# The first eight attention units: scores in banks of their own, computed two units ahead, with fills of 512 columns of zeros

## The chip, the cores and the metric

The kernel runs on one core of a Trainium2 chip. The metric is the device time of one execution in microseconds (us), the median of several runs; lower is better. The engines are TensorE (PE, with its weight loads as PEld), VectorE (DVE), ScalarE (ACT), GpSimd (POOL) and SyncE (SP), which here only issues DMAs.

## What is computed

Three layers follow one another. The first is local attention over 4 batches, 8 heads, 768 tokens and a head size of 64; the other two are gated feed-forward layers over the 3072 resulting rows of 512 numbers.

```python
for c in range(nc):                       # 24 chunks of 32 queries
    k_full = np.concatenate([mem_k, k_ctx], axis=2)   # 8 + up to 56 keys
    v_full = np.concatenate([mem_v, v_ctx], axis=2)
    scores = scale * np.matmul(q_c, k_full.transpose(0, 1, 3, 2))
    scores = scores - np.max(scores, axis=-1, keepdims=True)
    a = np.exp(scores)
    a = a / (np.sum(a, axis=-1, keepdims=True) + 1e-09)
    out[:, :, c_start:c_end] = np.matmul(a, v_full)
...
x = (1/(1+np.exp(-(x @ w_gate))) * (x @ w_val)) @ w_out       # 512 -> 1536 -> 512
h = x @ w_in                                                  # 512 -> 2048
g = (a0 + a1*h + a2*h**2 + a3*h**3) / (1 + |b0|*|h| + |b1|*h**2 + 1e-6)
y = g @ w_out
```

## The kernel before, in words

**Units.** The 768 tokens of a sequence are cut into 6 tiles of 128. A tile of one batch is a unit: 128 queries of 8 heads. The first eight units (two tiles of four batches) are computed before any feed-forward work exists. The later units are mixed into feed-forward products and are not touched by the change, apart from names.

**One unit g.** Five steps follow each other, and each waits for the one before:

1. `scores(g)`, TensorE: 32 small matmuls of q and k into two of the four banks of `ps_h` (`ps_att[g % 2]`).
2. `softmax(g)`, VectorE: a row maximum, and scores minus maximum into `probs`. `exp_scores(g)`, ScalarE, in place. `normalize(g)`, VectorE: (in the first tile a small memset,) row sum, plus 1e-9, reciprocal, multiplication.
3. `turn(g)`, TensorE: four transposes, again into `ps_att[g % 2]`; `copy_turned(g)`, ScalarE, to `probs_t`.
4. `weigh_values(g)`, TensorE: 32 small matmuls with v, again into `ps_att[g % 2]`.
5. `stage_x(g)`, ScalarE: out of `ps_att[g % 2]` to `x_raw`, and the semaphore `x_staged`.

All three matmul steps of a unit use the same two banks, so `scores(g)` waits for `stage_x(g-2)`. Every fp32 matmul is two matmul records in the trace; the fp32r matmuls of the feed-forward part are one.

**Order.** All order is written out by hand, engine by engine. `attention(first, fill)` goes through pairs of units; `fill(p, place)` or `at(p, place)` puts other work between the steps. On TensorE this other work is `warm_up(n)`, n products of the identity with itself into a bank of `ps_y` that nobody reads, and towards the end `early_product(c, m)`, the first products of the feed-forward layer. On ScalarE and VectorE it is the splitting of weights (`split_w(c, i)`) and of x (`split_x`) into a high and a low part for fp32r products, each time the high part on ScalarE first, then the low part on VectorE. VectorE also makes `token_sum(T1..T4, g)`, differences of parts of x. After unit 7, `last_operands` makes the last sums and splits: `token_sum(T3, 0)`, `(T4, 0)`, three splits and `split_w(1, 3)`, then `token_sum(T1, 1)` and `(T2, 1)`, which need the last staging.

**Loads.** SyncE issues them in order. `load_qk(g)` (q 256 KB, k 368 KB) writes one of two buffers and waits for `scores(g-2)`; `load_v(g)` (512 KB) waits for `weigh_values(g-2)`; `load_raw(c)` (512 KB) brings gate and value weights, from which GpSimd makes four sums. A load that waits holds back all loads behind it.

## Time and profile before

| | before |
|---|---|
| median of 3 runs | 1165.22 us (1165.1 to 1166.02) |
| the profiled execution | 1163.57 us |
| its span | 1161.6 us |
| TensorE busy | 1145.8 us (99%) |
| VectorE busy | 926.5 us (80%) |
| ScalarE busy | 750.9 us (65%) |
| GpSimd busy | 123.3 us (11%) |

The durations in the text come from the profiled execution. Its own time is 1.97 us more than its span, and 1.65 us under the median. "Busy" of TensorE counts its fills too, and a matmul record lasts longer than the time until the next one may follow.

### The profile page before, as it was taken

What the parts mean: (1) busy time and instruction counts of PE and PEld (TensorE: products, weight loads), DVE (VectorE), ACT (ScalarE), POOL (GpSimd) and SP (SyncE); (2) the same over time, 40 slices, a digit from 0 to 9 for tenths busy, and PEclk for the clock granted to TensorE, in tenths of its full rate; (3) what the DMA queues carried; (4) which work ended last, traced back from release to release, by engine and by line L of the source; (5) the groups of instructions that cost most, each with busy time, mean ns of one, the idle gap of its engine ahead of it and who ended that gap; (6) DMA issues with size and microseconds to landing.
All of it is one profiled execution on the core that took longest, in us unless ns stands there. A gap on an engine that the chain in (4) does not pass through costs nothing.

```text
span 1161.6 us, 20825 instructions
## 1 busy us (share of the span) xinstructions
PE 1145.8 (99%) x7954; PEld 942.8 (81%) x7954; DVE 926.5 (80%) x1419; ACT 750.9 (65%) x1224; POOL 123.3 (11%) x150
## 2 busy tenths in 40 slices
PE   7899999999999999999999999999999999999998
PEld 6788887778888777888888888888888888888887
DVE  5886767776676777777667998988988988988987
ACT  3665555455555555555556877877877877877875
POOL 2052230012233001223100000000000000000000
PEclk9999999999999999999999999999999999999999
DMA  7511412742141374323137100200200200200100
GB/s 261 165 64 55 163 55 95 230 149 91 60 157 55 100 234 158 109 86 105 46 129 264 42 1 1 73 1 1 72 0 0 72 0 0 72 0 0 37 1 37
DMA packets 40720, 94.05 MB, mean 81 GB/s; under 512 B 4288, under 2 KB 4288, under 8 KB 40640
## 3 DMA queue, kind: packets, MB, share of 16 engines
q1 hardware_dynamic: 40640, 92.95, 23.7%
q8 instruction: 54, 0.88, 0.3%
q14 instruction: 26, 0.21, 0.1%
HBM read 80.35 MB, written 12.58 MB: 80 GB/s over the span
## 4 chain that ended last, share of the span: by engine, by line
PE 94%; DVE 3%; issue 1%; DMA 1%; ACT 0%; SPq 0%; POOL 0%; ACTq 0%; POOLq 0%; DVEq 0%
PE ps_h L1253 9%; PE ps_h L1255 9%; PE ps_h L1260 9%; PE ps_h L1417 7%; PE ps_h L1412 7%; PE ps_h L1413 7%; PE ps_y L1456 7%; PE ps_y L1452 7%; PE ps_y L1450 7%; PE ps_y L1332 5%; PE ps_y L1337 5%; PE ps_y L1333 4%; PE ps_h L1235 2%; PE ps_h L1211 2%; PE ps_y L1321 1%
## 5 line engine op out<-in xcount | busy, mean ns | idle before, releaser
L1253 PE MATMUL ps_h<-xop,wop 128*128 128x512 f32 x484 | 188.3, 389 | 0.0
L1255 PE MATMUL ps_h<-xop,wop 128*128 128x512 f32 x484 | 188.3, 389 | 0.0
L1412 PE MATMUL ps_h<-x_split,weights 128*128 128x512 f32 x384 | 149.4, 389 | 0.0
L1413 PE MATMUL ps_h<-x_split,weights 128*128 128x512 f32 x384 | 149.4, 389 | 0.0
L1260 PE MATMUL ps_h<-xop,wop 128*128 128x512 f32 x484 | 149.0, 389 | 0.0
L1450 PE MATMUL ps_y<-weights,hid 128*128 128x512 f32 x360 | 140.0, 389 | 0.0
L1452 PE MATMUL ps_y<-weights,hid 128*128 128x512 f32 x360 | 140.0, 389 | 0.0
L878 DVE TENSOR_TENSOR wop<-rawp,wop 128x448 fp32r<-128x448 f32 x144 | 91.1, 661 | 32.7 <-ACT wop L494 32.7
L757 ACT ACTIVATE tmp<-ps_h 128x512 f32<-128x512 f32 x96 | 57.2, 595 | 92.4 <-PE ps_h L1417 92.4
L899 DVE TENSOR_TENSOR x_raw<-ps_h,probs_t 128x512 f32<-128x512 f32 x70 | 48.1, 687 | 79.6 <-PE ps_h L1260 79.3
L1332 PE MATMUL ps_y<-hid,wout 128*128 128x512 f32 x264 | 105.7, 400 | 0.6 <-DVE stage_h L930 0.3
L1253 PEld LDWEIGHTS ps_h<-xop,wop 128*128 128x128 f32 x484 | 90.8, 188 | 18.9
L1260 PEld LDWEIGHTS ps_h<-xop,wop 128*128 128x128 f32 x484 | 90.9, 188 | 18.9
L1255 PEld LDWEIGHTS ps_h<-xop,wop 128*128 128x128 f32 x484 | 90.8, 188 | 18.8
L1333 PE MATMUL ps_y<-hid,wout 128*128 128x512 f32 x264 | 103.1, 391 | 0.0
L1417 PE MATMUL ps_h<-x_split,weights 128*128 128x512 f32 x384 | 102.6, 389 | 0.0
L1456 PE MATMUL ps_y<-weights,hid 128*128 128x512 f32 x360 | 96.2, 389 | 0.0
L1130 DVE TENSOR_TENSOR tmp<-tmp 128x512 f32<-128x512 f32 x96 | 66.1, 689 | 30.8 <-ACT tmp L760 30.7
L535 ACT ACTIVATE hid<-x_raw 128x512 fp32r<-128x512 f32 x72 | 45.4, 631 | 63.4 <-DVE x_raw L913 63.4
L1413 PEld LDWEIGHTS ps_h<-x_split,weights 128*128 128x128 f32 x384 | 72.1, 188 | 15.0
L1417 PEld LDWEIGHTS ps_h<-x_split,weights 128*128 128x128 f32 x384 | 72.1, 188 | 14.9
L1412 PEld LDWEIGHTS ps_h<-x_split,weights 128*128 128x128 f32 x384 | 72.0, 188 | 14.9
(103 smaller groups left out, 2277.9 us busy)
## 6 DMA issues: line engine op xcount, KB each, us to landing
rawp<-wgv_l SPq DMA_DIRECT2D x36, 512.0 KB, 3.8
oraw<-wo_l SPq DMA_DIRECT2D x72, 256.0 KB, 3.9
unit<-v_l SPq DMA_DIRECT2D x24, 512.0 KB, 4.5
unit<-k_l SPq DMA_DIRECT2D x24, 368.0 KB, 4.2
unit<-q_l SPq DMA_DIRECT2D x24, 256.0 KB, 3.4
x_stage<-y_dram SPq DMA_DIRECT2D x6, 1024.0 KB, 5.7
out<-stage SPq DMA_DIRECT2D x24, 256.0 KB, 2.3
braw<-wb_l SPq DMA_DIRECT2D x11, 512.0 KB, 5.6
```

Source lines behind the costliest of these rows:

```text
L878: nc.vector.tensor_tensor(wop[:, c % 2, 1, cols], rawp[:, c % 2, 256 + 448 * i:256 + 448 * (i + 1)], wop[:, c % 2, 0, cols].bitcast(F32), ...
L1253: nc.tensor.matmul(dst, w_h[k], xop[:, m, 0, k, :], start=first and k == 0, stop=False, skip_group_check=True)
L1255: nc.tensor.matmul(dst, w_l[k], xop[:, m, 0, k, :], start=False, stop=False, skip_group_check=True)
L1260: last = nc.tensor.matmul(dst, w_h[k], xop[:, m, 1, k, :], start=False, stop=k == 1, skip_group_check=True)
L1332: nc.tensor.matmul(ps_y[:, m, :], w_at(0, m), h[0], start=f == 0, stop=False)
L1333: nc.tensor.matmul(ps_y[:, m, :], w_at(1, m), h[0], start=False, stop=False)
L1412: nc.tensor.matmul(dst, lhs(c, 0), x_split[:, 0, c, :], start=(c == 0), stop=False)
L1413: nc.tensor.matmul(dst, lhs(c, 1), x_split[:, 0, c, :], start=False, stop=False)
L1417: last = nc.tensor.matmul(dst, lhs(c, 0), x_split[:, 1, c, :], start=False, stop=(c == KT - 1))
L1450: nc.tensor.matmul(ps_y[:, m, :], hid_b(i, 0)[:, P * m:P * (m + 1)], wb_at(i, 1, 0), start=(i == 0), stop=False)
L1452: nc.tensor.matmul(ps_y[:, m, :], hid_b(i, 0)[:, P * m:P * (m + 1)], wb_at(i, 1, 1), start=False, stop=False)
L1456: nc.tensor.matmul(ps_y[:, m, :], hid_b(i, 1)[:, P * m:P * (m + 1)], wb_at(i, 1, 0), start=False, stop=False)
```

## The change

Only the first eight units are concerned.

- Their scores go to `ps_y` (`ps_first`), which is free at that time. Turned probabilities and outputs stay in `ps_att`. `scores(g)` of these units waits for `shifted` (the subtraction of unit g-2) instead of `x_staged`.
- Scores are computed two units ahead: `first_attention` replaces `attention(0, ...)` on TensorE, ScalarE and VectorE. Row maxima get a tile of their own (`row_maxima`), since the maximum of unit g+2 is now taken near the row sums of unit g.
- A fill is one product of the identity with 512 columns of zeros (`wide_fill`) into a bank of `ps_att` that holds nothing then, instead of `warm_up(3)` of 128 columns into `ps_y`. GpSimd zeroes the tile of zeros after the identity.
- SyncE asks for q and k of unit 2 right after those two of units 0 and 1 and V of unit 0, and so on.
- `split_w` and `split_x` have new places in the list.

```diff
-WARM = 3
+WARM = 6
...
+        ps_first = [ps_y[:, 0:2, 0:256], ps_y[:, 2:4, 0:256]]
...
-            for g in range(2):
+            load_qk(0)
+            load_qk(1)
+            load_v(0)
+            load_qk(2)
+            load_v(1)
+            load_qk(3)
+            load_raw(0)
+            for g in range(4, UNITS):
                 load_qk(g)
-            for g in range(2):
-                load_v(g)
-            load_raw(0)
-            load_qk(2)
-            for g in range(3, UNITS):
-                load_qk(g)
-                if g == 3:
+                load_v(g - 2)
+                if g == 4:
                     load_raw(1)
-                load_v(g - 1)
+            load_v(UNITS - 2)
             load_v(UNITS - 1)
```

VectorE, in place of `attention(0, at_start)`:

```diff
+            def first_attention():
+                softmax(0)
+                softmax(1)
+                for g in range(UNITS):
+                    normalize(g)
+                    if g == 2:
+                        split_w(0, 0)
+                    elif g == 3:
+                        split_w(0, 1)
+                    elif g == 4:
+                        split_w(0, 3)
+                        split_x(0, B11)
+                    elif g == 5:
+                        split_x(0, B21)
+                    elif g == 6:
+                        token_sum(0, T1, 0)
+                        token_sum(0, T2, 0)
+                        split_w(1, 2)
+                    if g + 2 < UNITS:
+                        softmax(g + 2)
+                    if g == 3:
+                        split_w(0, 2)
+                    elif g == 4:
+                        split_w(1, 0)
+                    elif g == 5:
+                        split_w(1, 1)
```

ScalarE, in place of the same call:

```diff
+                exp_scores(0)
+                exp_scores(1)
+                for g in range(UNITS):
+                    copy_turned(g)
+                    if g + 2 < UNITS:
+                        exp_scores(g + 2)
...
+                    stage_x(g)
+                    if g == 1:
+                        split_w(0, 0)
+                    elif g == 2:
+                        split_w(0, 1)
+                        split_w(0, 2)
+                    elif g == 3:
+                        split_x(0, B11)
+                        split_w(0, 3)
+                        split_w(1, 0)
```

TensorE:

```diff
                 if n >= 2:
-                    pe.wait_ge(x_staged, g - 1)
+                    if s:
+                        pe.wait_ge(x_staged, g - 1)
+                    else:
+                        pe.wait_ge(shifted, g - 1)
...
+            def wide_fill(b):
+                nc.tensor.matmul(ps_h[:, 2 * b, :], ident[:], zeros[:], start=True, stop=True)
...
+            def first_attention():
+                scores(0)
+                pe.wait_ge(ident_done, 3)
+                wide_fill(0)
+                scores(1)
+                for g in range(UNITS):
+                    if 1 <= g < UNITS - 2:
+                        scores(g + 2)
+                    turn(g)
+                    if g:
+                        pe.wait_ge(x_staged, g)
+                    if g == UNITS - 1:
+                        early_product(1, M1)
+                    else:
+                        wide_fill((g + 1) % 2)
+                    weigh_values(g)
+                    if g == 0:
+                        scores(2)
+                    elif g == UNITS - 2:
+                        early_product(0, M1)
+                        early_product(0, M2)
+                    else:
+                        wide_fill((g + 1) % 2)
+                early_product(1, M2)
```

**TensorE, the start of the program.** `ident` by `ident` is a warm-up, `unit` 32x64 are scores, `ident,probs` are the turns, `probs_t,unit` is the weighing of values. Before:

```order
L1242 MATMUL ps_y<-ident 128x128 x6
L1211 MATMUL ps_h<-unit 32x64 x32
L1242 MATMUL ps_y<-ident 128x128 x3
L1211 MATMUL ps_h<-unit 32x64 x32
L1242 MATMUL ps_y<-ident 128x128 x2
L1221 MATMUL ps_h<-ident,probs 128x128 x4
L1242 MATMUL ps_y<-ident 128x128 x3
L1235 MATMUL ps_h<-probs_t,unit 64x32 x32
L1242 MATMUL ps_y<-ident 128x128 x3
L1211 MATMUL ps_h<-unit 32x64 x32
L1221 MATMUL ps_h<-ident,probs 128x128 x4
L1242 MATMUL ps_y<-ident 128x128 x3
```

And now, where `zeros,ident` is a wide fill:

```order
L1235 MATMUL ps_y<-unit 32x64 x32
L1272 MATMUL ps_h<-zeros,ident 128x512
L1235 MATMUL ps_y<-unit 32x64 x32
L1247 MATMUL ps_h<-ident,probs 128x128 x4
L1272 MATMUL ps_h<-zeros,ident 128x512
L1261 MATMUL ps_h<-probs_t,unit 64x32 x32
L1235 MATMUL ps_y<-unit 32x64 x64
L1247 MATMUL ps_h<-ident,probs 128x128 x4
L1272 MATMUL ps_h<-zeros,ident 128x512
L1261 MATMUL ps_h<-probs_t,unit 64x32 x32
L1272 MATMUL ps_h<-zeros,ident 128x512
```

Scores of unit 2 stand behind the weighing of unit 0 in both, but those of unit 3 now follow them at once, and from there on two sets of scores are ahead of the turn. Each product of these rows is two records in the trace, a turn is one.

**VectorE, the start of the program.** A reduce of `ps` with a subtraction is a softmax, the memset to the multiplication is a normalize. Before:

```order
L817 TENSOR_REDUCE row_stats<-ps_h 128x8
L820 TENSOR_TENSOR probs<-ps_h,row_stats 128x2x4x64
L830 MEMSET probs 32x8x16
L835 TENSOR_REDUCE row_stats<-probs 128x8
L837 TENSOR_SCALAR row_stats<-row_stats 128x8
L839 RECIPROCAL row_stats<-row_stats 128x8
L841 TENSOR_TENSOR probs<-probs,row_stats 128x2x4x64
L817 TENSOR_REDUCE row_stats<-ps_h 128x8
L820 TENSOR_TENSOR probs<-ps_h,row_stats 128x2x4x64
L830 MEMSET probs 32x8x16
```

And now:

```order
L827 TENSOR_REDUCE row_maxima<-ps_y 128x8
L830 TENSOR_TENSOR probs<-ps_y,row_maxima 128x2x4x64
L827 TENSOR_REDUCE row_maxima<-ps_y 128x8
L830 TENSOR_TENSOR probs<-ps_y,row_maxima 128x2x4x64
L840 MEMSET probs 32x8x16
L845 TENSOR_REDUCE row_stats<-probs 128x8
L847 TENSOR_SCALAR row_stats<-row_stats 128x8
L849 RECIPROCAL row_stats<-row_stats 128x8
L851 TENSOR_TENSOR probs<-probs,row_stats 128x2x4x64
L827 TENSOR_REDUCE row_maxima<-ps_y 128x8
L830 TENSOR_TENSOR probs<-ps_y,row_maxima 128x2x4x64
```

The softmax of unit 1 moved ahead of normalize(0), and the softmax of unit 2 ahead of normalize(1).

**SyncE, the loads, with what each waits for.** From the load of q of unit 1 on. Before:

```order
L262 DMA unit<-q_l 128x512
L263 DMA unit<-k_l 128x736
L268 DMA unit<-v_l 128x1024 x2
L274 DMA rawp<-wgv_l 128x1024
L262 DMA unit<-q_l 128x512 [waits scores_done]
L263 DMA unit<-k_l 128x736
L262 DMA unit<-q_l 128x512 [waits scores_done]
L263 DMA unit<-k_l 128x736
L274 DMA rawp<-wgv_l 128x1024
L268 DMA unit<-v_l 128x1024 [waits pv_done]
```

And now:

```order
L266 DMA unit<-q_l 128x512
L267 DMA unit<-k_l 128x736
L272 DMA unit<-v_l 128x1024
L266 DMA unit<-q_l 128x512 [waits scores_done]
L267 DMA unit<-k_l 128x736
L272 DMA unit<-v_l 128x1024
L266 DMA unit<-q_l 128x512 [waits scores_done]
L267 DMA unit<-k_l 128x736
L278 DMA rawp<-wgv_l 128x1024
L266 DMA unit<-q_l 128x512 [waits scores_done]
L267 DMA unit<-k_l 128x736
```

V of unit 1 and the first weights (`rawp`) now stand behind a load that waits for scores; before, they were issued at once.

## Rows read from the trace of the kernel before

**Rows 1.** Windows view, core 0: length, then PE, PEld, DVE, ACT, POOL busy, clock, DMA, GB/s

```profile
5.76:54.11 48.35, 40.47 (x1110) 34.73 (x1110) 39.21 (x72) 23.19 (x40) 6.18 (x8) 0.96 0.64 220
...
57.00:1161.00 1104.00, 1099.12 (x6761) 902.63 (x6759) 885.08 (x1344) 723.87 (x1179) 116.41 (x136) 1.00 0.22 74
...
20.28:23.70 3.42, 3.42 (x77) 3.13 (x75) 2.54 (x4) 1.92 (x5) 0.47 (x1) 0.52 0.71 215
```

**Rows 2.** Waits of VectorE, 5.7 to 54.2 us: total us, times, longest

```profile
DVE row_stats L817 <- PE ps_h L1211: 10.6, 5, 5.8
DVE probs L830 <- ACT probs L456: 2.0, 4, 0.7
DVE wop L878 <- ACT wop L494: 0.7, 1, 0.7
DVE row_stats L835 <- ACT probs L456: 0.3, 2, 0.2
```

**Rows 3.** Timeline of VectorE: start, us, engine, line, operation, idle before

```profile
5.76 0.69 DVE L817 TENSOR_REDUCE row_stats<-ps_h 128x8 f32<-128x512 f32 x1 [5.76 <-PE ps_h L1211]
6.49 0.69 DVE L820 TENSOR_TENSOR probs<-ps_h,row_stats 128x512 f32<-128x512 f32 x1
7.92 0.17 DVE L830 MEMSET probs<- 32x128 f32 x1 [0.74 <-ACT probs L456]
...
9.28 0.69 DVE L841 TENSOR_TENSOR probs<-probs,row_stats 128x512 f32<-128x512 f32 x1
...
53.42 0.69 DVE L858 TENSOR_TENSOR t_raw<-x_raw 128x512 f32<-128x512 f32 x1
```

**Rows 4.** Timeline of TensorE, units 1 and 2

```profile
7.69 0.85 PE L1211 MATMUL ps_h<-unit 64*32 64x64 f32 x64 [0.59 <-DMA unit<-k_l]
...
10.03 0.66 PE L1221 MATMUL ps_h<-ident,probs 128*128 128x128 f32 x4 [0.84 <-DVE probs L841]
...
11.42 1.13 PE L1235 MATMUL ps_h<-probs_t,unit 64*64 64x32 f32 x62
13.61 0.30 PE L1235 MATMUL ps_h<-probs_t,unit 64*64 64x32 f32 x2 [1.07 <-issue]
13.84 0.94 PE L1242 MATMUL ps_y<-ident 128*128 128x128 f32 x6
14.71 0.86 PE L1211 MATMUL ps_h<-unit 64*32 64x64 f32 x64
15.50 0.66 PE L1221 MATMUL ps_h<-ident,probs 128*128 128x128 f32 x4
15.99 0.83 PE L1242 MATMUL ps_y<-ident 128*128 128x128 f32 x6
16.89 0.89 PE L1235 MATMUL ps_h<-probs_t,unit 64*64 64x32 f32 x45
19.16 0.54 PE L1235 MATMUL ps_h<-probs_t,unit 64*64 64x32 f32 x19 [1.38 <-issue]
```

**Rows 5.** Waits of TensorE, 4 to 54.5 us

```profile
PE ps_h L1235 <- issue: 3.0, 3, 1.4
```

**Rows 6.** Timeline of TensorE in the stretch of low clock

```profile
21.60 1.11 PE L1221 MATMUL ps_h<-ident,probs 128*128 128x128 f32 x4
22.51 1.48 PE L1242 MATMUL ps_y<-ident 128*128 128x128 f32 x6
```

**Rows 7.** Timeline of TensorE, unit 6 and first products

```profile
44.81 1.14 PE L1235 MATMUL ps_h<-probs_t,unit 64*64 64x32 f32 x64
...
46.44 0.40 PE L1253 MATMUL ps_y<-xop,wop 128*128 128x512 f32 x1
46.67 0.39 PE L1255 MATMUL ps_y<-xop,wop 128*128 128x512 f32 x1
```

**Rows 8.** Page, DMA queues: packets, MB, share of 16 engines

```profile
q8 instruction: 54, 0.88, 0.3%
```

**Rows 9.** Groups of ScalarE by line and shape, 4 to 54.5 us

```profile
L472 ACT ACTIVATE x_raw<-ps_h 128x512 f32<-128x512 f32 x8 | 4.8, 595 | 8.9 <-PE ps_h L1235 8.9
```

More of the change, by code:

```diff
@@ L114, in build @@
         ps_att = [ps_h[:, 0:2, 0:256], ps_h[:, 2:4, 0:256]]
+        ps_first = [ps_y[:, 0:2, 0:256], ps_y[:, 2:4, 0:256]]
         probs = [probs_all[:, b, :].rearrange("p (h s k) -> p h s k", h=HP, s=2) for b in range(2)]
         probs_t = [probs_t_all[:, b, :].rearrange("p (h n) -> p h n", h=HP) for b in range(2)]
-        row = [row_stats[:, b].rearrange("p (s h) -> p s h", s=2) for b in range(2)]
+        row, row_max = [[x[:, b].rearrange("p (s h) -> p s h", s=2) for b in range(2)] for x in (row_stats, row_maxima)]
         NQC, NKC, NVC = HP * P, CT * HP * KEYS, CT * HP * D
@@ L432, in _ @@
                                     pattern=[[-1, P]], channel_multiplier=1).then_inc(ident_done, 1)
+            nc.gpsimd.memset(zeros[:], 0.0).then_inc(ident_done, 1)
             def weight_sums(c):
@@ L814, in softmax @@
                 b = g % 2
-                sc = ps_att[b].rearrange("p s (h k) -> p s h k", k=KEYS)
+                sc = (ps_first if g < UNITS else ps_att)[b].rearrange("p s (h k) -> p s h k", k=KEYS)
                 dve.wait_ge(scores_done, g + 1)
-                nc.vector.tensor_reduce(row[b], sc, AX.X, ALU.max).then_inc(max_done, 1)
+                nc.vector.tensor_reduce(row_max[b], sc, AX.X, ALU.max).then_inc(max_done, 1)
                 dve.wait_ge(max_done, g + 1)
@@ L820, in softmax @@
                 nc.vector.tensor_tensor(probs[b].rearrange("p h s k -> p s h k"), sc,
-                                        row[b].unsqueeze(3).to_broadcast([P, 2, HP, KEYS]),
+                                        row_max[b].unsqueeze(3).to_broadcast([P, 2, HP, KEYS]),
                                         ALU.subtract).then_inc(shifted, 1)
@@ L1196, in scores @@
                 b, s, n = g % 2, g // UNITS, g % UNITS
+                dst = (ps_att if s else ps_first)[b]
                 pe.wait_ge(qk_loaded[b], 32 * (g // 2 + 1))
                 if n >= 2:
[L1199 removed]
+                    if s:
+                        pe.wait_ge(x_staged, g - 1)
+                    else:
+                        pe.wait_ge(shifted, g - 1)
                 elif s and n == 0:
@@ L1238, in weigh_values, with warm_up @@
                 last.then_inc(pv_done, 1)
-            def warm_up(products):
+            def warm_up(products, b=0):
                 for _ in range(products):
-                    nc.tensor.matmul(ps_y[:, 3, 0:P], ident[:], ident[:], start=True, stop=True)
+                    nc.tensor.matmul(ps_att[b][:, 0, 0:P], ident[:], ident[:], start=True, stop=True)
+            def wide_fill(b):
+                nc.tensor.matmul(ps_h[:, 2 * b, :], ident[:], zeros[:], start=True, stop=True)
             def product(c, m):
@@ L1345, in attention @@
                     scores(a)
-                    if b == 1:
-                        warm_up(WARM)
-                        scores(b)
                     if p:
@@ L1354, in attention @@
                     fill(p, 1)
-                    if b > 1:
-                        scores(b)
+                    scores(b)
                     if p == 0:
@@ L1366, in attention, with first_attention @@
                 fill(UNITS // 2, 1)
-            def fill_first(p, place):
-                if (p, place) == (3, 4):
-                    early_product(0, M1)
-                    early_product(0, M2)
-                elif (p, place) == (4, 0):
-                    early_product(1, M1)
-                elif (p, place) == (4, 1):
-                    warm_up(WARM)
-                    early_product(1, M2)
-                elif place != 2:
-                    warm_up(1 if p == 0 and place < 2 else WARM)
+            def first_attention():
+                scores(0)
[8 more added lines that the diff above has]
+                        pe.wait_ge(x_staged, g)
+                    if g == UNITS - 1:
+                        early_product(1, M1)
[10 more added lines that the diff above has]
+                early_product(1, M2)
             pe.wait_ge(ident_done, 2)
-            warm_up(2 * WARM)
-            attention(0, fill_first)
+            warm_up(WARM)
+            first_attention()
             for s in range(NS):
```

67 lines of the change are left out of this document (19 added, 48 removed).

## The prediction, made blind

> **What bounds the kernel now.** The windows view comes first. From 57 us to 1161 us TensorE is busy for 1099.12 of 1104 us [rows 1], so nothing there is shortened by this change. What the change touches lies ahead of that point; it can only move the moment at which the dense part begins.
>
> In the first 57 us I looked for an engine that does the same work before and after and sits on the path. That is VectorE. Its work from the first row maximum (5.76) to the last sum that the late operands need, `token_sum(T2,1)` (starts 53.42, 0.69 long, so it ends at 54.11) [rows 3], is the same set of instructions in both kernels; only their order differs. ScalarE's split of that sum, and behind it the dense product chain, hang on it. So the question is: how long does VectorE stand idle in this stretch, before and after?
>
> Before: the stretch is 48.35 us and VectorE is busy for 39.21 [rows 1]. Its waits are 10.6 less the 5.8 ahead of the first instruction, 2.0, 0.7 and 0.3, that is 7.8 us [rows 2]; the remaining 1.3 us are the small gaps between instructions. The largest part, 4.8, is waiting for scores, so TensorE is late. It is late for a reason of its own: it stops inside runs of matmuls that wait for no other engine. Weighing the values alone stops three times, 3.0 us, as "issue" [rows 5]. Between two such stops (13.61 and 19.16) stand 2+6+64+4+6+45 = 127 matmul records [rows 4]; with their weight loads 254 instructions, with two semaphore instructions 256. The instruction queue moved 54 packets with 0.88 MB, 16.3 KB each [rows 8], which is 256 instructions of 64 bytes. I read this as instruction fetch: blocks of 256 come one at a time, and late when TensorE eats small matmuls fast. The block from 13.61 to 19.16 took 5.5 us, 1.38 of them standing still [rows 4].
>
> **What the change does, part by part.** I go through VectorE's new order and add up its idle time.
>
> *Wait for the scores of unit 1.* VectorE now does two softmaxes first. It is done with the first at 6.49+0.69 = 7.18 [rows 3]. Scores of unit 1 used to start at 7.69, when their K had landed, and took 0.85 [rows 4], so VectorE would wait 1.4. V of unit 1 and the first weights, which shared the queues with this load, now go out behind a wait, so K should land earlier; with the fill ahead of the scores ending near 7.0 the wait is 0.7 at least. I take 0.9. What goes away is the wait for the exponential at the small memset, 2.0 us in four places [rows 2], since another softmax now stands between.
>
> *Wait for the scores of unit 2.* This is the largest term. VectorE does normalize(0), then softmax(2). TensorE does turn(0), fill, weigh(0), and only then scores(2). From the end of normalize: 0.05 until the turn; 1.39 from the start of the turn to the start of weighing (10.03 to 11.42) [rows 4]; weighing 1.14 with the tail of its last record, 1.07 until the next may follow [rows 7]; scores 0.86 [rows 4] and 0.03 until VectorE starts. Together 3.4 us, 3.3 to 3.6, in which VectorE has nothing to do. Before, normalize(1) filled that hole.
>
> *Fills.* An old one is three products, six records; a new one is one product of 512 columns, two records. Six records of 128 columns take 0.83, each following the last by some 0.11 [rows 4]. A record of 512 columns in the fp32r form follows by 0.23 (46.44 to 46.67) [rows 7]. So a new fill costs between 2 x 0.23 = 0.46, if each record passes its columns once, and 4 x 0.22 = 0.89, if an fp32 record costs twice its columns, as 0.11 against a quarter of 0.23 says. I take 0.89. The fill between turn and weighing is free either way: four turns of 0.11 and 0.89 make 1.33, under the 1.39 that the copy between them takes anyway. The one behind weighing costs its 0.89, 0.2 more than the old one.
>
> *Pace afterwards.* TensorE per unit: scores 0.79 (14.71 to 15.50) [rows 4], turn to weighing 1.39, weighing 1.07, fill 0.89, together 4.1. VectorE per unit: softmax 1.42, normalize 2.05 (7.92 to 9.97) [rows 3], so 3.5, and from unit 2 on some 8 us of splits and sums spread over five units. So VectorE is as slow as TensorE or slower, unless TensorE stops. A unit has 64+64+4+4 = 136 records (144 before), still about one fetch per unit. Counted on from the first stop of before, which stood behind record 222, blocks now end behind scores(4), in scores(5), (6) and (7), and in weigh(6). The stop behind scores(4) delays turn(2), and VectorE may not overwrite those probabilities before it: 1.3, about the 1.38 of the row. The next costs 0.3; the later ones fall while VectorE has splits to do. I take 1.6, with 0.3 (only the 0.3 is left) and 2.8 (twice a stop of 1.4) as bounds.
>
> *Splits.* split_w(0,0) on VectorE now stands behind normalize(2). ScalarE can deliver it at 1.39 + 1.14 + 0.05 + 0.60 for staging [rows 9] + 0.6 for its own half, 3.8 us behind the start of turn(1); VectorE wants it at 0.7+0.7+2.05 = 3.5. So it waits 0.3. The same holds for two more, one of them behind a longer split: 1.2 together, at least 0.5.
>
> *Tail.* turn(7) now stands behind weigh(6) and two products, twelve records at 0.23 (2.7 us), while its normalize is long done. The last staging then comes late for VectorE by 0.5, between 0 and 1.0.
>
> Sum: 0.9 + 3.4 + 1.6 + 1.2 + 0.5 = 7.6 us idle, against 7.8. What is gained late in the phase is paid for by the hole at its beginning.
>
> *Clock.* In the stretch 20.28 to 23.70 the granted clock was 0.52 [rows 1], that is the 1.2 GHz level; just before it TensorE had stood still for 1.38. At this level the turn took 1.11 and the fill 1.48 [rows 6], against 0.66 and 0.83 [rows 4]. In the new order TensorE stands still for longer than anywhere before: from about 7.9 to 11.6 ahead of turn(0), and some 2.8 us ahead of turn(1). If the clock falls there it costs 0.45 on the turn, part of 0.89 on the fill and 0.2 on weighing, 1.5 in all if it covers them. I take 0.9 for one fall that covers them in part, and 1.9 as the bound.
>
> The Trainium skill, "TensorE: Matmul & The Clock Gate" (Why this matters for your kernels), warns of idle gaps between bursts of matmuls, since they bring the lower clock back. This rule speaks against the change; the trace agrees as far as its one fall stands behind a stop.
>
> So idle is 8.5 against 7.8, and the dense part starts 0.8 later in round numbers (the terms are rounded to 0.1). The profiled execution took 1163.57 (1161.6 of span and 1.97 around it) and becomes 1164.4. The median of the runs shown is 1165.22, 1.65 above it, and I put the forecast on the median: **1166.0**. About 0.2% (2.3 us) is what a measurement of this kernel can tell from no change.
>
> **Rivals.**
> *Faster (0.17).* Fetches arrive while TensorE waits for normalize anyway, the clock stays up, and K of unit 1 lands early: idle 0.7 + 3.3 + 0.3 + 0.6 + 0.2 = 5.1, 2.7 less than before, 1162.5. For it speaks that the DMA engines are used for only 0.64 of the stretch [rows 1], so that a fetch need not queue. Against it: the hole of 3.3 stays in every case, and so the other terms must nearly vanish together.
> *Slower (0.27), the clock.* Place: turn(0) to weigh(0) and turn(1) to weigh(1), both behind 2.8 us or more in which TensorE has nothing to do. If the clock falls both times and covers both, that is 3.0 on top of 7.6, 2.8 later, 1168.0. It decides when both stretches run at 1.2 GHz; with one of them the time stays within 0.2%. Against it: TensorE stopped several times before, and the clock fell once.
> *The fills cost half (0.04).* With 0.46 each TensorE reaches the end of a block sooner and waits there longer, by about as much as it saves: 1165.6.
> *No fetch stops (0.05).* If a whole phase fitted into the instruction memory, the stops would be something else, tied to the old order, and could be gone: 8.5 less 1.6, 0.9 less than before, 1164.3.
> *The forecast (0.47).* Idle within 1.5 us of 8.5: 1164.5 to 1167.4.
>
> The Trainium skill, "Advanced Engine Details and Errata" (ISA Cache), gives lines of 16 KB, 256 instructions, as the packets here have, but 128 KB in all for TensorE. By that size fetches could run far ahead, as in the case without fetch stops; the stops inside runs of matmuls speak against it.
>
> **Range.** Low bounds together: 0.7+3.3+0.3+0.5+0 = 4.8, 3.0 less than before: 1162.2. High bounds: 1.4+3.6+2.8+1.2+1.0+1.9 = 11.9, 4.1 more: 1169.3. I take 1162.8 to 1169.0. Faster 0.17; within 0.2% 0.56 (the forecast, the cheap fills, no fetch stops); slower 0.27.
>
> **What would show it.** In the profile of the changed kernel VectorE's reduction of unit 2 waits 3.3 to 3.6 us for scores, that of unit 1 0.7 to 1.4; the two records of a wide fill follow each other by 0.44 at full clock; stops of TensorE stand 127 records apart, the first between scores(4) and turn(2); token_sum(T2,1) ends near 54.9. The prediction is wrong if the scores of unit 2 come before 14.0, if the stops vanish, or if TensorE stays at 1.2 GHz over several stretches.

## The result: 7 us slower

The changed kernel takes 1172.98 us (median of 6 runs, 1171.06 to 1176.52), the one before 1165.94 (6 runs, 1165.1 to 1167.1): a ratio of 1.0066, with an interval of 1.0053 to 1.0078, so 7.0 us more. A second session gave 1172.24 against 1165.38, 1.0053 [1.0033 to 1.0073]. The forecast was 1166.0, with 1169.0 as the upper end of its range. The profiled execution took 1173.7 us.

The windows view of the changed kernel, cut at VectorE's first row maximum and at the end of `token_sum(T2,1)` (length, then PE, PEld, DVE, ACT, POOL busy, clock, DMA share, GB/s):

```profile
5.83:61.14 55.31, 45.35 (x1044) 29.25 (x1044) 38.27 (x72) 23.19 (x40) 6.04 (x8) 0.81 0.59 198
61.14:1171.60 1110.46, 1102.31 (x6770) 905.00 (x6768) 886.41 (x1348) 726.33 (x1183) 117.25 (x136) 1.00 0.22 74
```

VectorE runs the same 72 instructions as before [rows 1], but the stretch is 55.31 us instead of 48.35, and it ends 7.03 later. What lies behind it, 1110.46, was 1107.49 in the single profile of before. Over the kernels of this study this second part lies between 1107.5 and 1113.1 in the profiled executions, 1107.5 to 1110.4 in the old order and 1108.1 to 1113.1 in the new one, so I take most of those 3.0 us for scatter, which isn't shown: the medians differ by 7.0, as the first part does, while these two profiled executions differ by 10.1.

Waits of VectorE in that stretch (total us, times, longest; the first line holds the 5.83 ahead of the stretch):

```profile
DVE row_maxima L827 <- PE ps_y L1235: 15.7, 5, 5.9
DVE wop L888 <- ACT wop L501: 3.4, 3, 1.9
DVE probs L830 <- PE ps_h L1247: 1.1, 2, 0.7
DVE x_raw L863 <- ACT x_raw L479: 0.7, 1, 0.7
DVE xop L880 <- ACT xop L491: 0.6, 1, 0.6
```

That is 9.9 + 3.4 + 1.1 + 0.7 + 0.6 = 15.7 us of waiting, against 7.8 [rows 2] and the 8.5 of the forecast. The wait for the exponential is gone, as expected. Where the new ones stand is in its timeline:

```profile
8.54 0.69 DVE L827 TENSOR_REDUCE row_maxima<-ps_y 128x8 f32<-128x512 f32 x1 [1.29 <-PE ps_y L1235]
17.86 0.69 DVE L827 TENSOR_REDUCE row_maxima<-ps_y 128x8 f32<-128x512 f32 x1 [5.89 <-PE ps_y L1235]
27.20 0.66 DVE L888 TENSOR_TENSOR wop<-rawp,wop 128x448 fp32r<-128x448 f32 x1 [1.92 <-ACT wop L501]
29.19 0.69 DVE L827 TENSOR_REDUCE row_maxima<-ps_y 128x8 f32<-128x512 f32 x1 [1.34 <-PE ps_y L1235]
35.52 0.69 DVE L827 TENSOR_REDUCE row_maxima<-ps_y 128x8 f32<-128x512 f32 x1 [1.38 <-PE ps_y L1235]
```

The largest part of the excess is in one row: the scores of unit 2 are waited for 5.89 us, where 3.3 to 3.6 were forecast. TensorE's timeline shows what it did meanwhile:

```profile
12.03 1.11 PE L1247 MATMUL ps_h<-ident,probs 128*128 128x128 f32 x4 [3.53 <-DVE probs L851]
12.94 1.92 PE L1272 MATMUL ps_h<-zeros,ident 128*128 128x512 f32 x2
14.78 1.93 PE L1261 MATMUL ps_h<-probs_t,unit 64*64 64x32 f32 x64
16.64 2.05 PE L1235 MATMUL ps_y<-unit 64*32 64x64 f32 x128
21.35 1.11 PE L1247 MATMUL ps_h<-ident,probs 128*128 128x128 f32 x4 [2.66 <-DVE probs L851]
22.26 1.91 PE L1272 MATMUL ps_h<-zeros,ident 128*128 128x512 f32 x2
```

It stood still for 3.53 us, and then turn, fill, weighing and scores ran at the lower clock: the turn takes the 1.11 of [rows 6], the weighing 1.86 to the next row instead of 1.07. The windows view gives the clock:

```profile
8.60:10.00 1.40, 0.00 (x0) 0.00 (x0) 1.37 (x3) 0.01 (x1) 0.00 (x0) 1.00 0.92 341
10.10:30.50 20.40, 15.81 (x339) 10.59 (x340) 9.73 (x21) 4.79 (x9) 6.04 (x8) 0.50 0.63 218
30.60:61.00 30.40, 27.00 (x639) 17.52 (x638) 25.40 (x47) 17.55 (x31) 0.00 (x0) 1.00 0.51 163
```

From 10.1 to 30.5 us, three units long, TensorE has the 1.2 GHz level (0.50), and before and behind it 2.4 GHz. It fell while TensorE stood still ahead of turn(0). Before, the low stretch was 3.4 us long [rows 1]. One of the prediction's own signs of being wrong is thus there: TensorE stays at 1.2 GHz over several steps and units.

In the low stretch TensorE has no stop for issue. Behind it there are three, 3.1 us together, inside `scores(5)`, `scores(6)` and, not shown, `scores(7)`:

```profile
33.34 0.77 PE L1235 MATMUL ps_y<-unit 64*32 64x64 f32 x55
35.14 0.32 PE L1235 MATMUL ps_y<-unit 64*32 64x64 f32 x9 [1.02 <-issue]
...
38.95 0.71 PE L1235 MATMUL ps_y<-unit 64*32 64x64 f32 x46
40.69 0.41 PE L1235 MATMUL ps_y<-unit 64*32 64x64 f32 x18 [1.02 <-issue]
```

### The profile page after: what moved, and what is told of

It is laid out like the page before. It is cut to its first block, busy times and chain, and to the rows that moved or that the text cites. A ratio compares the mean times of both kernels' runs of the same rounds, so it can differ in the third digit from the quotient of the medians.

```text
span 1171.6 us, 20696 instructions
## 1 busy us (share of the span) xinstructions
PE 1151.8 (98%) x7888; PEld 938.0 (80%) x7888; DVE 924.7 (79%) x1419; ACT 750.8 (64%) x1224; POOL 124.5 (11%) x151
## 4 chain that ended last, share of the span: by engine, by line
PE 94%; DVE 3%; DMA 1%; issue 1%; SPq 0%; ACT 0%; ACTq 0%; DVEq 0%
PE ps_h L1283 9%; PE ps_h L1285 9%; PE ps_h L1290 9%; PE ps_h L1457 7%; PE ps_h L1453 7%; PE ps_h L1452 7%; PE ps_y L1496 7%; PE ps_y L1492 7%; PE ps_y L1490 7%; PE ps_y L1362 5%; PE ps_y L1367 5%; PE ps_y L1363 4%; PE ps_h L1261 2%; PE ps_y L1351 1%; PE ps_h L1247 1%; PE ps_h L1235 1%
```

## Experiments

Each kernel ran several times beside the kernel before. The last four columns are in us and come from the one profiled execution. T2 is the start of `token_sum(T2,1)`. "Waits" are VectorE's, from its first row maximum to the end of that sum. "At 1.2" is the time at the lower clock ahead of T2. "Issue" is what TensorE's waits put down to issue from 4 us to the end of T2. A 0.001 of the ratio is 1.2 us.

| kernel | median us | ratio, interval | T2 | waits | at 1.2 | issue |
|---|---|---|---|---|---|---|
| before | 1165.94 | | 53.42 | 7.8 | 3.4 | 6.0 |
| changed | 1172.98 | 1.0066 [1.0053, 1.0078] | 60.45 | 15.7 | 20.5 | 3.1 |
| scores(2) early | 1169.59 | 1.0033 [1.0021, 1.0046] | 57.26 | 12.1 | 6.8 | 5.7 |
| fills in the waits | 1169.75 | 1.0034 [1.0021, 1.0047] | 57.14 | 11.6 | 0 | 5.9 |
| narrow fills | 1169.22 | 1.0022 [1.0007, 1.0037] | 56.33 | 11.9 | 13.7 | 0.5 |
| before, wide fills | 1166.91 | 1.0005 [0.9989, 1.002] | 55.80 | 9.9 | 3.4 | 6.2 |
| before, new loads | 1169.75 | 1.0027 [1.0009, 1.0045] | 59.82 | 13.7 | 13.7 | 7.3 |
| three of them together | 1168.39 | 1.0026 [1.0012, 1.0041] | 58.43 | 12.7 | 10.2 | 5.6 |
| fills not of zeros | 1173.21 | 1.0068 [1.0044, 1.0092] | 60.23 | 15.8 | 10.2 | 3.1 |
| fills in the waits, half the weighing | 1163.57 | 0.9979 [0.9965, 0.9993] | 52.94 | 7.5 | 0 | 0 |
| old loads | 1170.67 | 1.0048 [1.0031, 1.0064] | 57.56 | 12.7 | 13.7 | 2.5 |
| fills in the waits, old loads | 1168.23 | 1.0025 [1.0014, 1.0036] | 57.58 | 12.3 | 0 | 6.1 |
| three together, old loads | 1171.58 | 1.0052 [1.0035, 1.0069] | 62.30 | 17.4 | 20.5 | 3.7 |
| before, half the weighing | 1162.32 | 0.9975 [0.9961, 0.9989] | 48.94 | 3.1 | 0 | 1.8 |
| changed, half the weighing | 1167.23 | 1.001 [0.9993, 1.0026] | 53.76 | 8.9 | 3.4 | 0 |
| before, new loads, half the weighing | 1169.14 | 1.0015 [0.9996, 1.0034] | 56.46 | 11.4 | 6.8 | 6.8 |
| before, new loads, split moved | 1168.5 | 1.0031 [1.0016, 1.0046] | 54.40 | 8.9 | 6.8 | 5.4 |
| old loads, again | 1171.39 | 1.0047 [1.0029, 1.0066] | 59.20 | 14.5 | 17.1 | 1.6 |
| changed, again | 1172.24 | 1.0053 [1.0033, 1.0073] | 60.82 | 15.7 | 20.5 | 3.3 |

The profiled execution is one of several, and not always near the median: that of "split moved" took 1165.08, that of "three together, old loads" 1178.21.

### The clock: fills in the waits

```diff
                 scores(1)
+                for _ in range(4):
+                    wide_fill(1)
                 for g in range(UNITS):
                     if 1 <= g < UNITS - 2:
                         scores(g + 2)
+                    if g == 1:
+                        for _ in range(3):
+                            wide_fill(1)
                     turn(g)
```

> Four more wide fills between scores(1) and turn(0), three more ahead of turn(1), so that TensorE does not stand still there. If idleness there brings the 1.2 GHz level (theory clock), the granted clock stays at 1.0 from 7 us on and the time is 1166 to 1168. If wide fills of zeros do not hold the clock (theory fills), it falls anyway and the time stays at 1172 to 1176. If the order alone is the cost, the gain is the share of the doubled durations only, 1170.

1.0034 against 1.0066 (1.0053 in the second session): 2 to 4 us of the 7 came back. That is less than the 1166 to 1168 expected with the clock held. The windows view of this kernel from the first row maximum to the end of T2:

```profile
5.87:57.83 51.96, 45.05 (x1058) 27.60 (x1058) 38.86 (x72) 23.27 (x40) 5.90 (x8) 1.00 0.62 211
```

And the waits of its VectorE in that stretch:

```profile
DVE row_maxima L827 <- PE ps_y L1235: 14.2, 5, 5.9
DVE wop L888 <- ACT wop L501: 1.2, 2, 1.0
DVE xop L880 <- ACT xop L491: 0.8, 1, 0.8
DVE x_raw L863 <- ACT x_raw L479: 0.7, 1, 0.7
DVE probs L830 <- PE ps_h L1247: 0.6, 1, 0.6
```

The clock is 1.00 throughout in this execution (over the whole execution the mean clock was 1.0 in six of the ten runs, 1168.7 to 1170.1, and 0.997 or 0.998 in four, 1170.8 to 1171.5). VectorE waits 8.3 + 1.2 + 0.8 + 0.7 + 0.6 = 11.6, which is 4.1 less than in the changed kernel. The hole ahead of the scores of unit 2 is 3.46, as forecast for the high clock. But with a faster TensorE the stops grew. Two of them in its timeline of TensorE, ahead of turn(1) and inside `scores(5)`:

```profile
17.82 2.41 PE L1272 MATMUL ps_h<-zeros,ident 128*128 128x512 f32 x5 [0.94 <-issue]
...
31.69 0.42 PE L1235 MATMUL ps_y<-unit 64*32 64x64 f32 x23 [1.59 <-issue]
```

And all waits of TensorE for issue up to 53 us:

```profile
PE ps_y L1235 <- issue: 5.0, 4, 1.6
PE ps_h L1272 <- issue: 0.9, 1, 0.9
```

5.9 us, against 3.1 in the changed kernel. The changed kernel has no such stop in its 20.4 us at 1.2 GHz, where this one has two (0.94 and 1.28). My reading is that at the low clock TensorE uses its instructions up more slowly, so that the next block is there in time, and part of what the clock costs is given back. That the stops are instruction fetch is borne out by the DMA view: in quarters of a us, one packet of the queue `q8 instruction` starts at 23.25, 29.25, 35.25 and 40.25, each 2.1 to 2.5 us ahead of the end of a stop (25.60, 31.69, 37.56, 42.60).

### The hole ahead of scores(2)

```diff
                 scores(1)
+                scores(2)
...
                     if g == 0:
-                        scores(2)
+                        pass
```

> Scores of unit 2 moved ahead of turn(0), the rest as in the changed kernel. If the hole in VectorE's order is the main cost (3.4 us at full clock, 5.9 as measured), the time falls to 1166 to 1168 and VectorE's reduction of unit 2 waits for nothing. If the low clock is the main cost and comes from TensorE standing still ahead of turn(0), it stays still for some 1.5 to 2.5 us there, the clock may fall all the same, and the time is 1169 to 1171.

1.0033, in the 1169 to 1171 of the second case. The reduction of unit 2 no longer waits, but other waits of TensorE took its place:

```profile
10.72 0.85 PE L1235 MATMUL ps_y<-unit 64*32 64x64 f32 x64 [1.94 <-DMA unit<-k_l]
12.31 0.66 PE L1247 MATMUL ps_h<-ident,probs 128*128 128x128 f32 x4 [0.74 <-DVE probs L851]
24.89 0.66 PE L1247 MATMUL ps_h<-ident,probs 128*128 128x128 f32 x4 [3.13 <-issue]
29.96 0.32 PE L1235 MATMUL ps_y<-unit 64*32 64x64 f32 x9 [0.72 <-issue]
```

K of unit 2 lands at 10.7, and a stop of 3.13 stands ahead of turn(2), for which VectorE waits 3.17. The time is 2.3 to 3.8 us under that of the changed kernel, and part of that is clock: two low stretches of 3.4 us in its profile, from 12.9 and from 36.8 us, and not 20.4.

### The fills

In the new order, `warm_up(3, b)` (three products of 128 columns) in place of each wide fill; in the kernel before, one product with 512 columns of zeros in place of each `warm_up(3)`; and in the changed kernel another number in the tile:

```diff
-            nc.gpsimd.memset(zeros[:], 0.0).then_inc(ident_done, 1)
+            nc.gpsimd.memset(zeros[:], 0.7310585).then_inc(ident_done, 1)
```

> The changed kernel with each wide fill replaced by three products of the identity with itself, as before. Theory clock (idleness): the clock falls at turn(0) as before, within 1 us of 1173. Theory fills (zeros or width do not hold the clock, or cost time): it recovers sooner, 1167 to 1170.

> The kernel before with every fill of three products replaced by one wide fill of zeros, nothing else. Theory fills: the clock is low for many us in the first phase and the time is 1169 or more. Theories order and clock by idleness: within 1.5 us of before, since each fill costs 0.2 us more and most lie beside a wait.

> The changed kernel with 0.7310585 in place of the zeros that the wide fills stream. If zeros do not count as activity for the clock, the stretch at 1.2 GHz shrinks from 20 us to 3 or 7 and the time is 1168 to 1170. If only being busy counts, nothing changes: 1172 to 1174.

1.0022, 1.0005 and 1.0068. In the order of before, wide fills make no difference that can be measured, as expected (within 1.5 us). In the new order narrow ones give back 3.6 to 5.1 us (1.0022 against 1.0053 and 1.0066), at least as much as fills in the waits do. This is the "theory fills" of the first expectation (1167 to 1170) and not its "theory clock" (within 1 of 1173). In the profile the clock falls all the same, at 11.8, and TensorE is at 1.2 GHz for 13.7 us. But it hardly stops for issue any more:

```profile
PE ps_h L1247 <- DVE probs L851: 8.7, 4, 3.5
...
PE ps_h L1268 <- issue: 0.5, 1, 0.5
```

So the kind of fill is part of the loss. Whether it works through their own length, the clock or the stops wasn't separated. A wide fill takes 1.84 at the low clock (12.94 to 14.78), more than the 0.60 of the copy behind which it was to hide, and 1.06 behind a weighing at the high one (32.28 to 33.34 in the changed kernel), where 0.89 was forecast. What the fill holds makes no difference to the time, as the second case of the last expectation has it: 1.0068 against 1.0066.

The profile of the third holds something more. It was at 1.2 GHz for 10.2 us, half as long as the changed kernel, and its VectorE waited just as long (15.8). In the place of the low clock there is one stop between `scores(4)` and `turn(2)`:

```profile
28.01 0.66 PE L1247 MATMUL ps_h<-ident,probs 128*128 128x128 f32 x4 [3.13 <-issue]
```

Less low clock alone thus doesn't bring the time back. The eleven runs of the changed kernel say the same: three with a mean clock of 0.998 or 0.999 took 1170.4 to 1172.8 us, five with 0.990 or 0.991 took 1172.2 to 1176.5.

### The stops: half the weighing left out

```diff
-                        for e in range(2):
+                        for e in range(1 if g < UNITS - 1 else 2):
```

This leaves out 32 of 64 records in each of the weighings of units 0 to 6, so that TensorE has fewer instructions to fetch. The output is another. It was done in the kernel with fills in the waits, in the kernel before, and in the changed kernel. The expectations take each weighing to become 0.5 us shorter by it, but it doesn't. With fills in the waits the weighing of unit 0 takes 1.06 us to the next row with 64 records and 1.05 with 32:

```profile
13.69 1.14 PE L1261 MATMUL ps_h<-probs_t,unit 64*64 64x32 f32 x64
14.75 1.51 PE L1235 MATMUL ps_y<-unit 64*32 64x64 f32 x128
...
13.43 1.12 PE L1261 MATMUL ps_h<-probs_t,unit 64*64 64x32 f32 x32
14.48 1.55 PE L1235 MATMUL ps_y<-unit 64*32 64x64 f32 x128
```

So at the high clock leaving them out changes the number of instructions and not the length of the weighing, and what it gives back is the stops.

> As b_fill_holes, but units 0 to 6 leave out half of the 32 matmuls that weigh the values (the second head of each pair). Theory fetch: 104 instead of 136 records in a unit, so fewer blocks are fetched in the same stretch and TensorE's stops fall from 5.9 us to under 2; together with the shorter weighing (0.5 us a unit, on the path in unit 0 alone) token_sum(T2,1) ends 3 to 5 us earlier than the 57.8 of b_fill_holes, time 1164 to 1167. If the stops are not fetch, they stay and the gain is 0.5 to 1.5.

> The kernel before, units 0 to 6 leaving out half of the matmuls that weigh the values. Theory fetch: the stops (6 us in the trace) go here too, and token_sum(T2,1) ends 3 to 5 us before 54.1, time 1160 to 1163. If only the new order is bound by fetch, the gain is the shorter weighing alone, half a us for each unit, 1162 to 1164, with the stops still there.

> The changed kernel as it is, with its own fills, but units 0 to 6 leave out half of the matmuls that weigh the values (so its output is another). With the clock held by fills in the holes the same cut gave 1163.6 (ratio 0.9979), and it took all issue waits away. Theory (two separate causes, the clock and the fetch): no issue waits here either, but the clock still falls ahead of turn(0) or turn(1), and with it the time lies above 1163.6 by what the low stretches cost, 1 to 4 us: 1164.6 to 1167.6, ratio 0.999 to 1.0015. Rival (the low clock is a consequence of the fetch stops): without stops the clock stays up and the time is that of the kernel with fills in the holes, 1163 to 1164.

With fills in the waits the time fell from 1.0034 to 0.9979, 6.4 us, and TensorE has no wait for issue left. T2 ends 4.2 earlier, inside the 3 to 5 of theory fetch, and the time is a little under its 1164. In the kernel before the same change gave 0.9975, 2.9 us. That lies in both of its ranges, but T2 ends 4.5 earlier, and of 6.0 us of such waits 1.8 are left, which speaks for theory fetch. The window of the first, from the first row maximum to the end of T2:

```profile
5.74:53.63 47.89, 44.68 (x834) 27.31 (x834) 39.06 (x72) 22.96 (x40) 5.91 (x8) 1.00 0.67 229
```

Its waits of VectorE there:

```profile
DVE row_maxima L827 <- PE ps_y L1235: 10.5, 3, 5.7
DVE wop L888 <- ACT wop L501: 1.2, 2, 1.0
DVE x_raw L863 <- ACT x_raw L479: 0.7, 1, 0.7
DVE xop L880 <- ACT xop L491: 0.6, 1, 0.6
DVE probs L830 <- PE ps_h L1247: 0.2, 1, 0.2
```

And the window of the kernel before with half the weighing:

```profile
5.75:49.63 43.88, 37.98 (x886) 32.53 (x886) 39.34 (x72) 23.32 (x40) 6.12 (x8) 1.00 0.72 248
```

VectorE waits 4.8 + 1.2 + 0.7 + 0.6 + 0.2 = 7.5 us in the new order without stops and at the high clock. In the old order, with most stops gone, it is 43.88 - 39.34 = 4.5 idle in all, some 3.1 without the small gaps. So by VectorE the new order is 4.0 us worse still (T2 at 52.94 against 48.94), yet the medians are 1.3 us apart. VectorE's sum may be a good yardstick only as long as it is what is waited for last: in the old order with half the weighing the rest of the execution is 1159.6 - 49.63 = 1110.0 long, 2.5 more than before.

The third kernel tells whether the clock falls because of the stops. It has none (TensorE waits for VectorE, once for K, never for issue), but took 1.001, 3.6 us more than with fills in the waits, and its low stretch ahead of 60 us is this:

```profile
12.00:15.20 3.20, 3.20 (x22) 1.70 (x22) 0.00 (x0) 0.60 (x1) 0.00 (x0) 0.50 0.63 251
```

It stands behind 3.53 us of standing still ahead of turn(0), as in the changed kernel. The mean clock of its 12 runs is 0.991 to 0.999, that of the 10 runs with fills in the waits (and half the weighing) 1.0 in every run. Among the 12 the time goes with it: the four at 0.997 or above took 1165.0 to 1167.7, the six at 0.994 or below 1166.8 to 1170.9. So the clock is a cause of its own, as the theory said (ratio 0.999 to 1.0015).

### The order of the loads

Four kernels have only the loads exchanged: the kernel before with the new order, and the changed kernel, the one with fills in the waits, and a combination with the old one.

> The kernel before with the new order of loads alone. If the loads matter, K of unit 1 lands earlier than 7.69 us and the time falls by 0.5 to 1; but V of a unit is now asked for behind K and q of a later one. If the order of work and the fetch stops carry the loss, this stays within 1 us of before.

> The changed kernel with the loads in the order of before. f_loads_only showed the new order to cost 3 to 4 us in the kernel before. Theory loads: it gives 2 to 4 us back here too, 1169 to 1171. Theory compute order: the new order of work cannot use the old one (q and K of unit 5 now stand behind V of unit 4), so 1172 to 1174.

> b_fill_holes (clock held at 1.0) with the loads in the order of before. Loads work through the clock: with the clock held nothing is left of them, within 1 us of the 1169.75 of b_fill_holes. Loads work through longer fetches of instructions (data queued ahead of them): TensorE's stops change by 2 us or more, and the time by 1.5 or more.

New loads in the kernel before cost 1.0027, more than either expectation allowed. Its profile shows one stall: the first weights land at 16.6, since they are asked for behind `load_qk(3)`, and ScalarE, whose split of them stands ahead of the staging of unit 0, waits for them. ScalarE's timeline:

```profile
16.61 0.58 ACT L496 ACTIVATE wop<-rawp 128x448 fp32r<-128x448 f32 x1 [3.78 <-DMA rawp<-wgv_l]
17.09 0.58 ACT L474 ACTIVATE x_raw<-ps_h 128x512 f32<-128x512 f32 x1
```

TensorE's timeline names "issue" for the scores of unit 2, which by the code wait for that staging (`x_staged`, done at 17.67):

```profile
17.77 1.17 PE L1213 MATMUL ps_h<-unit 64*32 64x64 f32 x64 [2.38 <-issue]
```

In the changed kernel that split stands behind the staging of unit 1 and never waits for its weights. So I moved it in the kernel before with new loads too, and in another kernel I took the stops away instead:

```diff
-                if (p, place) == (0, 2):
+                if (p, place) == (0, 4):
                     split_w(0, 0)
```

> The kernel before with the new order of loads, and ScalarE's first half split of weights (0, 0) moved from ahead of the staging of unit 0 to behind it. With the new loads alone the profile shows that split waiting 3.8 us for its weights, and the staging of unit 0, for which the scores of unit 2 wait, stands behind it. Theory (the new order of loads costs through this queue alone): scores of unit 2 start near 15.6 instead of 17.8, and the ratio is 0.999 to 1.001. Rival (the order of loads costs by later data or by longer stops of TensorE, whatever ScalarE does): the ratio stays at 1.002 to 1.0035.

> The kernel before with the new order of loads, and units 0 to 6 leave out half of the matmuls that weigh the values (so its output is another). The new order of loads alone cost 1.0027; the same cut in the kernel before gave 1162.3 (0.9975). Theory (the order of loads costs because data then arrive while instruction fetches are due, which lengthens the stops): without stops the order of loads costs nothing, ratio 0.997 to 0.9985, 1162 to 1164. Rival (the order of loads costs because q, k or v themselves come late): the 3 to 4 us stay, ratio 1.000 to 1.0015, 1165.5 to 1167, with waits for DMA in the profile of TensorE and none for issue.

The reduction of unit 2 then came at 15.10 with a wait of 0.84 in the profile of the first, and its profiled execution took 1165.08. But its median over 11 runs is 1168.5, 1.0031, so my theory falls and the rival holds: that stall is in the profile, and removing it doesn't bring the time back. The second gave 1.0015, the upper end of the rival's range, where 0.997 to 0.9985 was the theory, with the same stall of ScalarE (4.2) and waits for V (2.3); stops for issue stayed too, so it doesn't separate the two as meant. New loads cost 3 to 5 us in the old order (1.0027, 1.0031, and 1.0015 against 0.9975), whatever was done beside them.

What goes with this cost is the clock. The median of the mean clock was 0.9945, 0.995 and 0.9965 in these three kernels, against 0.997 to 0.999 in the kernel before beside them, and their profiles have 13.7, 6.8 and 6.8 us at 1.2 GHz ahead of T2. In the kernel before itself, 110 runs over the sessions, those with a mean clock of 0.999 or more have a median of 1165.0 us and those with 0.996 or less one of 1169.7. A cost of 3 to 5 us is of that size. Why the clock falls more often with these loads isn't shown.

In the new order it is otherwise. Side by side in one session:

> The changed kernel with the old order of loads again (1.0048 before), now beside the changed kernel itself on one chip. Theory (the order of loads doesn't matter in the changed kernel; the two profiles had the same waits and stops up to 24 us, and differed by 13.7 against 20.5 us at the lower clock): the two ratios agree within 0.001, and both scatter with the clock. Rival (the old order of loads gives back 2 us): this one lies 0.002 under the other.

> The changed kernel as it is, beside the one with the old order of loads. Theory: 1.005 to 1.007, and within 0.001 of the other. Rival: 0.002 above the other.

1.0047 and 1.0053, 0.0006 apart; with fills in the waits, 1.0025 and 1.0034 in two sessions. Both differences are within the intervals, and the stops are nearly the same (6.1 against 5.9), so longer fetches aren't the way loads work there. The first session's 1170.67 alone had looked like 2 us given back. In its profile the waits of TensorE for VectorE (3.52, 2.66) and that of VectorE for the scores of unit 2 (5.89) are those of the changed kernel within 0.01; what differs is how long the clock stayed down. Its windows view:

```profile
10.50:24.00 13.50, 9.53 (x208) 6.21 (x212) 6.59 (x16) 2.94 (x5) 6.07 (x8) 0.50 0.57 208
24.20:58.00 33.80, 30.46 (x769) 19.88 (x762) 27.73 (x51) 18.99 (x33) 0.00 (x0) 1.00 0.58 183
```

13.5 us instead of 20.4, and T2 2.8 earlier. In the changed kernel the loads have no part that I could measure.

### Combinations

scores(2) early, narrow fills, and five and three of them in the waits:

> The changed kernel with scores of unit 2 ahead of turn(0), narrow fills of three products instead of wide ones, and two more stretches of narrow fills in the waits between the first three scores. Theory order plus clock: no hole and no stretch at 1.2 GHz after 7 us, so token_sum(T2,1) ends at 53 to 55 and the time is 1164 to 1166. Theory fetch: stops of TensorE take over what the hole gives back, token_sum(T2,1) ends at 55 to 57, 1166 to 1168.

> g_combined (scores of unit 2 early, narrow fills, fills in the waits) with the loads in the order of before: V of unit 1 and the first weights are asked for at once, so K of unit 2 lands later than 10.5 us. If the loads cost 3 us wherever they stand, 1165 to 1166, the best of the new orders and level with before; if K of unit 2 becomes the new wait, 1167 to 1169.

1.0026 (1168.39, above both ranges), no better than one of the parts alone, and with the old loads 1.0052 (1171.58, above both again): there K of the early scores is waited for (8.2 us, the longest 4.8), since it is asked for behind other loads. Here the clock fell too, at 14.0 and 12.1: the narrow fills don't close the waits, and TensorE had stood still for 1.47 and 1.29 in the first, and stood still in a wait of 4.76 in the second. Of the versions that do the whole work none beats the kernel before.

## Why the prediction was wrong, step by step

- **Place and yardstick: right, as far as one pair of profiles tells.** The loss of the medians is the one of the first 60 us, and VectorE's waits account for it: 15.7 - 7.8 = 7.9, less 0.9 that VectorE was busy for less (39.21 to 38.27), makes the 7.0.
- **The step that failed first is the clock term.** "I take 0.9 for one fall that covers them in part, and 1.9 as the bound." The mechanism was named, at the right place, and even as a rival (1168.0), but as falls that end with the weighing, 1.5 each, priced by turn, fill and weighing alone. The profile has one fall that lasts from 10.1 to 30.5, over three units with `scores(2)` to `scores(4)` in them. Holding the clock up takes 4.1 us of waiting from VectorE, and 3.7 us from the time by the ratios (1.0066 to 1.0034; 2.2 against the second session's 1.0053). What the sum lacked is that work goes on at the low clock and VectorE's next steps wait for it (0.67, 1.92, 1.34 in the rows behind the 5.89), and that the low stretch may be much longer than the 3.4 us of before. The one fall of before was also read too simply: it began at 20.28, and TensorE had run again since 19.16 [rows 4].
- **The stops: three positions of five right, price wrong.** They stand in scores(5), (6) and (7), and 127 records apart (9+4+2+64+2+46 from one to the next), as worked out; the one in weigh(6) isn't there. The one behind `scores(4)`, priced at 1.3 and so most of "I take 1.6", is missing in the changed kernel, which is at the low clock there. With a shorter low stretch it came and was 3.13, in two other kernels of this order. In the changed kernel the stops are 3.1, and at most one is passed on (1.38 ahead of the reduction of unit 5), inside the forecast. With the clock held they are 5.9, and leaving them out took VectorE's waits from 11.6 to 7.5, 4.1, above the 2.8 that was the bound: those in scores(4) and (5) are passed on to a reduction (1.46, 1.95), the last two fall while VectorE has splits to do, as forecast. The weighing is as long with half of its records, so the 4.1 is the stops' own.
- **The holes: right.** 3.46 for the scores of unit 2 at the high clock (3.3 to 3.6 forecast). For unit 1 the wait is 1.29, inside 0.7 to 1.4 but above the 0.9 taken: "K should land earlier" was wrong, scores(1) start at 7.65 instead of 7.69.
- **Splits and tail.** 1.2 and 0.7 at the high clock, with 0.6 more for a split of x, against 1.2 and 0.5. At the low clock the splits wait 3.4, because ScalarE's staging stands behind a slow weighing.
- **The wide fill.** Its cost was 0.89 forecast and 1.06 measured, and at 1.2 GHz it doesn't fit behind the copy: "free either way" held at the high clock only. That narrow fills would give back 3.6 to 5.1 us wasn't foreseen.
- **The loads** were taken at nothing in the changed kernel, which the last comparison doesn't contradict. It wasn't foreseen that they cost 3 to 5 us in the old order.

Taken away one after the other, the waits go from 15.7 to 11.6 with the clock held (4.1, where 0.9 was forecast) and to 7.5 with the stops left out too (4.1, where 1.6 was; 6.0 was forecast without either). These are steps of one path and not shares of the changed kernel. In it the stops are worth 1.4 at most by the rows, which would leave up to 6.8 of 15.7 - 7.5 = 8.2 for the low clock; holding the clock gives less back, because longer stops come in its place. This estimate rests on one profile of each.

The Trainium skill, "TensorE: Matmul & The Clock Gate" (Why this matters for your kernels), warns of idle gaps between bursts, since they bring the lower clock back. It was what spoke against the change, and the traces agree in the main. The clock fell between 10 and 13 us in the profiles of all six kernels of the new order that have no extra fills ahead of turn(0), and in the three with wide fills there it stayed up. In the two combinations, whose narrow fills left waits open, it fell too.

"Advanced Engine Details and Errata" (ISA Cache), also of the Trainium skill, has 128 KB for TensorE, by which fetches could run far ahead of stops such as those here. They came all the same, and went, or mostly went, with fewer records.

What stays open: why the new loads bring the clock down in the old order, by what the narrow fills help in the new one, why the clock returned after 13.5 us in one execution and after 20.5 in another with the same waits, and why leaving out half of the weighing gave 6.4 us by the ratios where VectorE's waits fell by 4.1.

## What to carry to other kernels

A reordering that opens a gap of a few microseconds ahead of TensorE has two prices, the gap and the clock behind it, and the second isn't bounded by the length of an earlier low stretch: price the whole dependent phase at the low clock. A third price can trade places with the second: at the high clock TensorE ran into longer stops, so take one of the two away and look at the other before you add them up. If a gap can't be avoided, try filling it; here seven wide fills in two gaps gave back a third to a half of the loss, and narrow fills in place of wide ones at least as much. Before work is put one engine ahead, list what was filling the hole (here the normalize of unit 1 ahead of the scores of unit 2), and when a wait is named "issue", look at what the instruction waits for in the code before it is read as a fetch.

## What the runs showed of the hardware

- The clock stayed at 1.2 GHz for 20.4 us in which TensorE was busy for 15.81. It came back when TensorE had run without a wait since 21.35; in an execution of the kernel with old loads, with the same waits, it came back after 13.5, TensorE having run since 21.14.
- In those 20.4 us TensorE had no stop for issue; at the high clock the same part of the program had two (0.94 and 1.28). In two executions that were at the high clock between `scores(4)` and `turn(2)` a stop of 3.13 stood there.
- Leaving out every second product of the weighing left it as long as it was, 1.05 us against 1.06, but took TensorE's 5.9 us of stops away.
- Fills of zeros and fills of 0.73 cost the same, 1.0066 and 1.0068.
